# A delta-rule attention and two mixtures on one core: gates, ids and weights of the first mixture moved ahead of its block, and one VectorE order changed inside it

## The reference

```python
for t in range(S):                       # delta rule, state 48 x 48 per head
    y[:, :, t] = einsum('bhd,bhde->bhe', q_t, state)
    v_old = einsum('bhde,bhd->bhe', state, k_t)      # k normalised
    state = state + beta_t * outer(k_t, v_t - v_old)

# mixture 1: eight experts, one per token, only where x @ w_skip > 0
e = argmax(x @ w_gate); g = softmax(x @ w_gate)[e]
out = x + g * (relu(x @ w1[e]) @ w2[e])              # 384 -> 1024 -> 384

# feed forward 2 ("second mixture" below), all tokens
out = relu(out @ w_in) ** 2 @ w_out                  # 384 -> 2048 -> 384
```

## Time and profile before

| | us |
|---|---|
| three runs | 1000.20, 1002.96, 998.68; median 1000.2 |
| profiled execution | 1002.22, of which span 1000.2 |
| PE busy / PEld busy | 910.4 / 830.8 (91% / 83% of the span) |
| DVE / ACT / POOL busy | 521.0 / 445.5 / 311.7 |
| mean granted clock of TensorE | 0.968 |

### The profile page before, as it was taken

The page is one execution under the profiler, slowest core; times in us unless marked ns, Lnnn a source line. Parts: engine busy times, 40 slices in busy tenths (PEclk is TensorE's granted clock), DMA queues, the critical chain, the costliest instruction groups (busy, mean ns, idle before and its releaser), DMA issues.

```text
span 1000.2 us, 27258 instructions
## 1 busy us (share of the span) xinstructions
PE 910.4 (91%) x11542; PEld 830.8 (83%) x11543; DVE 521.0 (52%) x974; ACT 445.5 (45%) x802; POOL 311.7 (31%) x306
## 2 busy tenths in 40 slices
PE   3899999999999972698999679999999999999998
PEld 3788888888888872688998559999999999999997
DVE  4466777768676642366677543334333333333332
ACT  4466666666666651344543533333233333332322
POOL 3456666575667642344553500000000000000000
PEclk9999999999999995799999969999999999999999
DMA  6243434433432311455546530020010010100100
GB/s 196 58 120 109 115 110 117 112 101 108 113 93 81 94 40 23 171 194 189 186 164 226 207 95 1 1 64 1 1 64 1 25 38 0 63 0 0 64 1 32
DMA packets 39063, 84.45 MB, mean 84 GB/s; under 512 B 9496, under 2 KB 29626, under 8 KB 36656
## 3 DMA queue, kind: packets, MB, share of 16 engines
q1 hardware_dynamic: 36016, 77.89, 24.7%
q0 software_dynamic: 2944, 5.05, 1.7%
HBM read 67.16 MB, written 17.42 MB: 85 GB/s over the span
## 4 chain that ended last, share of the span: by engine, by line
PE 50%; issue 5%; DMA 2%; DVE 2%; ACT 1%; POOL 0%; DVEq 0%; POOLq 0%; SPq 0%; ACTq 0%
PE h L1406 20%; PE acc L1422 20%; PE h L1330 5%; PE acc L1342 4%; DVE w_lo L1218 1%; PE t L1392 1%; DMA raw<-wts 1%; DVE hl L1230 0%; DMA rows_in<-x_rows 0%; ACT hh L1128 0%; DMA x_rows<-rows_out,scatter_ids 0%; DMA rows_in<-x_rows,gather_ids 0%; POOL rows_in L1042 0%; PE t L1317 0%; DVE xl L1275 0%
## 5 line engine op out<-in xcount | busy, mean ns | idle before, releaser
L1293 DVE SCALAR_TENSOR_TENSOR sqr<-h,relu 128x512 f32<-128x512 f32 x96 | 66.4, 692 | 185.1 <-ACT relu L1180 185.1
L1180 ACT ACTIVATE relu<-h 128x512 f32<-128x512 f32 x96 | 57.3, 597 | 193.4 <-PE h L1406 193.3
L586 DVE TENSOR_TENSOR X<-bX,cst 128x512 f16<-128x512 f32 x120 | 82.7, 689 | 94.6 <-PE bX L721 94.6
L1422 PE MATMUL acc<-w_hi,hh 128*128 128x384 f32 x384 | 129.5, 337 | 0.0
L1422 PE MATMUL acc<-w_hi,hl 128*128 128x384 f32 x384 | 129.3, 337 | 0.0
L1422 PE MATMUL acc<-w_lo,hh 128*128 128x384 f32 x384 | 129.0, 336 | 0.0
L1406 PE MATMUL h<-xh,w_hi 128*128 128x512 f32 x288 | 115.8, 402 | 1.4 <-DVE xl L1275 1.4
L1406 PE MATMUL h<-xl,w_hi 128*128 128x512 f32 x288 | 114.5, 398 | 0.0
L1406 PE MATMUL h<-xh,w_lo 128*128 128x512 f32 x288 | 114.3, 397 | 0.0
L1296 DVE TENSOR_TENSOR hl<-sqr,hh 128x512 fp32r<-128x512 f32 x96 | 66.5, 693 | 67.1 <-ACT hh L1182 67.1
L350 ACT ACTIVATE T<-bX 128x512 f16<-128x512 f32 x96 | 57.1, 595 | 87.6 <-PE bX L738 87.5
(11 more groups left out here) (157 smaller groups left out, 1942.4 us busy)
## 6 DMA issues: line engine op xcount, KB each, us to landing
raw<-wts SPq DMA_DIRECT2D x18, 1536.0 KB, 6.6
kq<-kqT SPq DMA_DIRECT2D x24, 448.0 KB, 4.2
R<-kv SPq DMA_DIRECT2D x24, 384.0 KB, 4.2
x_rows<-xs SPq DMA_DIRECT2D x48, 192.0 KB, 4.4
rows_in<-x_rows SPq DMA_DIRECT2D x8, 768.0 KB, 4.5
kn<-k_rows SPq DMA_DIRECT2D x24, 192.0 KB
out<-rows_out SPq DMA_DIRECT2D x24, 192.0 KB, 1.9
raw_w<-first_w SPq DMA_DIRECT2D x24, 128.0 KB
```

What stands on the lines that cost most here:

```text
L586: dve.tensor_tensor(of_blocks(X[:, lev], lev, 0), in_blocks(bX, lev), mask.unsqueeze(1).broadcast_to([P, H, *mask.shape[1:]]), ALU.mult).t ...
L1180: act.activation(relu[:, f % 2], hb[f % 2][:], ACT.Relu).then_inc(m_relu, 1)
L1293: dve.scalar_tensor_tensor(out=sqr[:, f % 2], in0=hb[f % 2][:], scalar=0.0, in1=relu[:, f % 2], op0=ALU.max, op1=ALU.mult).then_inc(m_sqr, 1)
L1422: last = pe.matmul(acc[sub][:, 0:DM], h[:, f % 4, sub * P:(sub + 1) * P], w[1][:, f // 8].rearrange("p (f d) -> p f d", f=8)[:, f % 8], st ...
```

## The change

In the first block:
- `Block(no_gpsimd_drain=True)`: GpSimd is not drained at its end.
- The last batch becomes two units (`UNITS`): pairs 20 to 22, marked and ranked in step 24, and pair 23 alone behind the last step. TensorE ranks the former in step 24, and waits in step 25 until VectorE has taken these ranks.
- Gates in two groups (`GATED`): pairs 0 to 19 with their first part in step 23, exp in step 24 and last part in step 24; pairs 20 to 23 at the end. Each group's gate is stored from this block.
- SyncE, in this block: `rc` is loaded early; expert 1's two weight halves behind steps 10 and 14; after both gate stores and when all ids are placed, the 256 ids of expert 0 alone (`gather_ids`).
- GpSimd clears `rows_in` at the start and issues expert 0's two gathers as its last act in the block.

In the second block SyncE starts with `first_ids`, GpSimd goes on to expert 1, and VectorE's order in a step is: ..., hl 2, hl 3, splits (1, 0) and (1, 1), xl of the next rows, split (1, 2), output rows.

```diff
+UNITS = [(m, 0, B) for m in range(BATCHES - 1)] + [(BATCHES - 1, 0, B - 1), (BATCHES - 1, B - 1, B)]
+GATED = [(0, PAIRS - B), (PAIRS - B, PAIRS)]
...
-        block = ctx.enter_context(nc.Block())
+        block = ctx.enter_context(nc.Block(no_gpsimd_drain=True))
...
             sp.dma_start(id_table.rearrange("(p c) o -> p (c o)", p=P), none[:]).then_inc(table_set, 16)
+            sp.dma_start(rc[:], rconst).then_inc(in_rc, 16)
...
+            def store_gates(k):
+                first, last = GATED[k]
+                sp.wait_ge(gate_ready, k + 1)
+                with nc.allow_non_contiguous_dma("one word of each row"):
+                    sp.dma_start(x_dram.rearrange("i p c -> p i c")[:, first:last, DM], gate[:, first:last])\
+                        .then_inc(gate_stored, 16)
...
+                if i in (10, 14):
+                    half = (i - 10) // 4
+                    sp.dma_start(raw[:, half], wts[1, half]).then_inc(w_in[half], 16)
 
             every_step(body)
+            for k in range(len(GATED)):
+                store_gates(k)
+            sp.wait_ge(ids_placed, 16 * PAIRS)
+            sp.dma_start(gather_ids[:, 0], id_table[0:BLOCK].rearrange("(p a) o -> p (a o)", p=P)).then_inc(first_ids_in, 16)
...
             pool.memset(none[:], NOWHERE).then_inc(none_set, 1)
+            pool.memset(rows_in[:], 0.0).then_inc(cleared, 1)
...
-            place_tokens(BATCHES - 1, range(B))
+            place_tokens(BATCHES - 1, range(B - 1))
+            place_tokens(BATCHES, (B - 1,))
+            pool.wait_ge(first_ids_in, 16)
+            pool.wait_ge(gate_stored, 16 * len(GATED))
+            for b in range(2):
+                pool.wait_ge(x_stored[b], 32 * (PAIRS // 2))
+            pool.wait_ge(cleared, 1)
+            pool.sem_inc(pool_moves, 1)
+            for a in range(2):
+                pool.indirect_dma_start(rows_in[:, 0, a * ROW:(a + 1) * ROW], None, x_dram.rearrange("i p c -> (i p) c"),
+                                        bass.IndirectOffsetOnAxis(ap=gather_ids[:, 0, a:a + 1], axis=0),
+                                        bounds_check=B * S - 1, oob_is_err=False).then_inc(gathered[0], 16)
...
+                if i == PAIRS:
+                    exponents(0)
                 from_x(0)
...
                 gram_drain(1)
+                if i == PAIRS:
+                    mark_best(BATCHES - 1)
+                    mark_ties(BATCHES - 1)
+                    mark_one(BATCHES - 1)
+                    take_ranks(BATCHES - 1)
+                    place_sums(BATCHES - 1)
+                    place_ids(BATCHES - 1)
+                    count(BATCHES - 1)
+                    gates_last(0)
...
+                if i == PAIRS - 1:
+                    gates_first(0)
...
+            mark_best(BATCHES)
+            mark_ties(BATCHES)
+            mark_one(BATCHES)
+            take_ranks(BATCHES)
+            place_sums(BATCHES)
+            place_ids(BATCHES)
+            gates_first(1)
+            count(BATCHES)
+            gates_last(1)
...
+                    if i > PAIRS:
+                        pe.wait_ge(rank_used, BATCHES)
...
                     from_chunk()
+                if i == PAIRS:
+                    pe.wait_ge(er_ready, i)
+                    rank(BATCHES - 1)
...
-            sp.wait_ge(gathered[0], 32)
-            load(1, 0)
-            load(1, 1)
...
                 hidden_lo(first, e, 2)
+                hidden_lo(first, e, 3)
                 split_lo(e + 1, 1 - par, 1, 0)
                 split_lo(e + 1, 1 - par, 1, 1)
-                hidden_lo(first, e, 3)
+                rows_lo(first, 1 - par, e + 1)
                 split_lo(e + 1, 1 - par, 1, 2)
-                rows_lo(first, 1 - par, e + 1)
```

More of the change, by code:

```diff
@@ L96, with delta_rule @@
 W_PART = 2 * HALF // PAIRS
[L99 to L100 removed]
+def delta_rule(nc, kqT, kv, k_rows, beta, w_route, consts, tokens, first_w, x_dram, x2_dram, id_table, wts, rconst, shared):
+    LG, gate, one_hots, w_hi, w_lo, raw, rows_in, rc, gather_ids, w_in, gathered, in_rc = shared
     ctx = ExitStack()
@@ L353, in _, with exponents @@
         def _(act):
+            def exponents(k):
+                of = slice(*GATED[k])
+                act.wait_ge(gated, 4 * k + 2)
+                act.activation(exps[:, of].rearrange("p i e -> p (i e)"), shifted[:, of].rearrange("p i e -> p (i e)"),
+                               ACT.Exp).then_inc(exp_done, 1)
             def squares(i, b, loads):
@@ L561, in place_ids @@
                     dve.wait_ge(in_cst, 48)
[L562 to L565 removed]
+                elif of.start == 0:
+                    dve.wait_ge(ids_placed, 16 * B * m)
+                dve.tensor_scalar(place_i[:, of], place[:, of], float(NOWHERE), None, ALU.add).then_inc(place_ready, 1)
+                if of.start == 0:
+                    dve.tensor_scalar(token[:], token[:], float(B * P), None, ALU.add).then_inc(place_ready, 1)
             def count(u):
[L569 removed]
+                of, n, marks = unit(u)
+                dve.tensor_reduce(added[:], one_hot[:, of].rearrange("p q e -> p e q"), AX_X, ALU.add).then_inc(counted, 1)
                 dve.wait_ge(counted, 1 + 2 * u + 1)
@@ L573, in count, with gates_first, gates_last @@
                 dve.tensor_copy(counts_h[:], one_hots[:]).then_inc(one_hot_ready, 1)
+            logits = LG[:].rearrange("p (i c) -> p i c", c=1 + E)[:, :, 1:]
+            def gates_first(k):
+                of = slice(*GATED[k])
+                dve.wait_ge(lg_drained, of.stop)
+                dve.tensor_reduce(largest[:, of], logits[:, of], AX_X, ALU.max).then_inc(gated, 1)
+                dve.wait_ge(gated, 4 * k + 1)
+                dve.tensor_tensor(shifted[:, of], logits[:, of], largest[:, of].unsqueeze(2).broadcast_to([P, of.stop - of.start, E]),
+                                  ALU.subtract).then_inc(gated, 1)
+            def gates_last(k):
+                of = slice(*GATED[k])
+                dve.wait_ge(exp_done, k + 1)
+                dve.tensor_reduce(largest[:, of], exps[:, of], AX_X, ALU.add).then_inc(gated, 1)
+                dve.wait_ge(gated, 4 * k + 3)
+                dve.tensor_scalar(largest[:, of], largest[:, of], 1e-9, None, ALU.add).then_inc(gated, 1)
+                dve.wait_ge(gated, 4 * k + 4)
+                dve.reciprocal(gate[:, of], largest[:, of]).then_inc(gate_ready, 1)
             def body(i):
@@ L877, in _, with feed_forward @@
             every_step(body)
-            rank(BATCHES - 1)
-def feed_forward(nc, wts, rconst, x_dram, x2_dram, id_table, out, shared):
-    one_hots, gate, w_hi0, w_lo0, ids_placed = shared
+            rank(BATCHES)
+def feed_forward(nc, wts, x_dram, x2_dram, id_table, out, shared):
+    one_hots, w_hi0, w_lo0, raw, rows_in, rc, gather_ids, w_in, gathered, in_rc = shared
     ctx = ExitStack()
@@ L978, in _ @@
         def _(sp):
-            sp.dma_start(rc[:], rconst).then_inc(in_rc, 16)
             def load(u, half):
                 sp.dma_start(raw[:, half], wts[u, half]).then_inc(w_in[half], 16)
-            with nc.allow_non_contiguous_dma("one word of each row"):
-                sp.dma_start(x_dram.rearrange("i p c -> p i c")[:, :, DM], gate[:]).then_inc(gate_stored, 16)
-            sp.wait_ge(ids_placed, 16 * B * BATCHES)
             sp.dma_start(first_ids[:], id_table.rearrange("(e r) o -> e (r o)", e=E)[:, 0:BLOCK]
                          .rearrange("e (p a) -> p e a", p=P)).then_inc(first_ids_in, 16)
-            sp.wait_ge(gathered[0], 32)
-            load(1, 0)
-            load(1, 1)
             sp.wait_ge(more_ready, 2)
@@ L1041, in _ @@
         def _(pool):
-            pool.memset(rows_in[:], 0.0).then_inc(cleared, 1)
             def split_lo(u, par, chunk):
```

129 lines of the change are left out of this document (53 added, 76 removed).

## The result

The changed kernel takes 993.5 us (median of ten runs, 989.5 to 997.2), the kernel before beside it 1002.7 (median of ten, 996.3 to 1004.6). The ratio, taken over all these runs, is 0.9926, with a 95% interval of 0.990 to 0.995 (the two medians alone give 0.991): faster, but by 9.2 us where 20.7 were forecast, and outside the range of 974 to 986. The profiled execution of the changed kernel took 989.46 us with a span of 987.7, that is 12.5 less than before's.

A forecast was written before the change was run, and what follows sets the result against it. TensorE is busy over 90% nearly throughout; the dips addressed were a serial latency thread before the first mixture and expert waits for hl. 1002.2 − 11.1 (transition) − 9.6 (experts) = 981.5, less 2.0 for the median: 979.5 us, range 974 to 986.

The forecast's parts named there:

- Routing, gates and exp ahead of the last logits: End of the recurrence: this work fits idle time of VectorE and ScalarE; nothing, at most 0.5 us without VectorE's cover.
- rival (e): ScalarE, recurrence's end: exp and table load need 2.7 to 3 us, making last logits 1.2 us later; 980.7, chance 0.1.
- Scatter landing 3.0, bound 4.5: Transition: the last position scatter lands 3.0 us after its start, with bounds of 2.2 and 4.5 us.
- rival (a): Transition: the ids load stays slow or the scatter lands late, giving 4 us back; 983.5, chance 0.2.
- Ids load 2.4: Transition: SyncE's load of 2 KB of ids takes 2.4 us, with bounds of 2.2 and 6.4 us.
- The drain 3.6 of the 11.1: End of first block: GpSimd's drain leaves the path, 3.6 us of the 11.1 us expected from the transition.
- Barrier and counts hidden: Start of second block: barrier, totals, thr and prefix sums end near 397, needed near 397.8; 0.8 us to spare.
- rival (c): Transition: barrier or new block's code comes late; only scatters and ids load are saved, 3.6 us fewer; 983, chance 0.1.
- Expert 1's weights: Recurrence: two 1.5 MB loads behind steps 10 and 14 delay only SyncE's queue; nothing, at most 1 us.
- Experts 9.6 less: Expert stage: 13.2 us of hl waits and slow clock go, 3.6 us charged for late xl; bounds 7.6 and 13.2.
- (b): Experts: GpSimd keeps the port or expert loads come late, gaining 5 us instead of 9.6; 984, chance 0.15.
- (d): Experts: late second weight half makes each step 21.7 us, so the kernel is slower; 1003.6, chance 0.04.

The follow-up runs named there:

- order_only: The kernel before with only VectorE's new order in the experts (hl 3 ahead of two splits, rows' low parts ahead of the last split): 992.0 us, ratio 0.986.
- hl_only: The changed kernel with hl 3 still ahead of the two splits, but the last split back ahead of the rows' low parts: one run of 1007.1 us.
- both: The changed kernel with 8 words of padding ahead of rows_out and expert 1's weights loaded behind the first gather: 981.7 us, ratio 0.979.
- late_weights: The changed kernel with expert 1's two weight loads back behind the first gather, as in the kernel before: 989.8 us, ratio 0.985.
- after_again: The changed kernel run once more, with nothing changed: 995.7 us, ratio 0.989 to the kernel before.

## Why the prediction was wrong, point by point

**Routing, gates and exp ahead of the last logits, cost nothing.** Right: exp ended before Ep was wanted, and step 24 is no longer than in order_only (12.3 us in both). The Trainium skill, ScalarE: Activation LUTs, section What ACT_TABLE_LOAD costs, has a drain beside the load; here exp starts 1.30 us after the load's start, so this trace shows no such drain, and rival (e) fell.

**Position 2.7 us after the logits, 0.87 more to the scatter, 0.95 and 1.35 to the gathers.** Right: 2.71 and 0.86, the first gather 0.93 after the ids, the second 1.34 behind it.

**Scatter landing 3.0, bound 4.5.** Wrong: 5.2, and 4.4 to 7.3 in the other profiles with the gates in the tail. I had set the gates' pieces against the load of the ids, not against the scatter, which goes out 4.7 us after them. This is the first half of rival (a). Without them it is 2.66, so the term was right for a queue at rest. **Ids load 2.4:** 1.7, smaller than its lower bound of 2.2. **Gather 3.03:** 3.5. Together the transition gave 9.3 instead of 11.1, so the term missed by 1.8; at the mean of the other profiles by some 3.

**The drain 3.6 of the 11.1.** As an item wrong: it is 1.4 once the gather is in front of it (and the items named there, 3.8, 3.6 and 4, already add up to 11.4). The total of the transition doesn't rest on it, since that was built up from the last logits on.

**Barrier and counts hidden.** Right, with 4.3 us to spare (397.3 to 401.6); rival (c) fell.

**Expert 1's weights "Nothing, at most 1 us".** Wrong, and the costliest: I asked only what data queue behind them in SyncE. The instruction queue's packets need the same DMA engines, and a late one goes with 2.35 us of idle time and then the lower clock, 7 us together. No row that I read of before shows it, since nothing so large is loaded in the recurrence. It isn't in the profile that the result came with, only in the median: some 4.5 us.

**Experts 9.6 less.** Right in size (10.0), and in the waits: no wait for hl is left of 11.5 us, 1.2 us of waits for xl stand in its place. In part it is right by the pair of moves only: the sum gives the gain to hl's place, and hl_only shows that this place alone brings nothing. Rivals (b) and (d) fell, though the second weight half keeps ScalarE waiting, 18.5 us in all.

**What no term had.** The second mixture, 3.1 us longer by the new addresses. I counted it at nothing without saying so. And the base: the forecast took 2.0 off for a median of 1000.2 of three runs; ten runs have 1002.7, so that 2.5 us of the gap are the base's.

The gap between 979.5 and 993.5 is 14.0 us: 2.5 base, 4.5 stall (an average over eight profiles), 3.1 tiles, 3 transition, less 0.4 for the experts, 12.7; the rest of 1.3 is within the interval of the ratio (2.6 us each way). That both comes 21.3 us below before, where 20.7 were forecast, doesn't confirm the sum: 5.1 us of it are the tiles' places, which no term had. Without the stall and with the changed kernel's tiles (late_weights) it is 13.2 us, and some 16 with the second mixture as it was.

## What to carry to other kernels

A large load moved "into idle time" shares the DMA engines with the packets of the instruction queue, and the same goes for thousands of small pieces and the small scatters that a serial thread waits for: ask what else is to be fetched or landed meanwhile, not only what is queued on the issuing engine. When a change moves allocations, compare the rate of a long untouched stage before and after: it can take or give more than the change itself. And when an operation is taken out from behind another, the wait moves to the next in line unless that one is moved too.

## What was not expected of the hardware

- TensorE can stop in the middle of a group of independent matmuls for 1.25 to 2.9 us while a 1.5 MB load fills the DMA engines (share 0.98), and its clock then stays at 0.50, for 12 us in after_again.
- Float32 matmuls with the same shapes go at 227 to 233 ns (512 columns) and 173.8 to 175.8 ns (384 columns) from one to the next, when nothing but the tiles' places changes.
- A scatter of 128 four-byte words to memory lands 2.7 us after its start at rest and up to 7.3 behind the 3072 four-byte pieces of the gates.
- The matmuls of the program's start run as slowly as at a granted clock of 0.50 (0.61 us for a group of eight, later 0.41) until some moment between 25 and 58 us that differs by execution, while the clock's column shows 1.00 throughout; the first logits move by 12 us with it.
